# An attention and two-MLP kernel: the up products of tile pairs as seven block products, and the first MLP for all tiles before the second

## The reference, cut to what matters

```
a   = softmax(normed k^T @ normed q / tau)         # 256 x 256, columns normed over 6016 tokens
x   = v @ a                                        # 6016 x 256
g, u = x @ w_gate, x @ w_val                       # 256 -> 1536 each
y   = (silu(g) * u) @ w_out                        # 1536 -> 256
h   = y @ w_in2                                    # 256 -> 2048
out = (h * clip(h + 3, 0, 6) / 6) @ w_out2         # 2048 -> 256
```

## Time and profile before

| what | us |
|---|---|
| median of 3 runs (lowest, highest) | 1154.29 (1154.23, 1155.18) |
| the profiled execution, its own time | 1154.73 |
| its span in the trace | 1152.9 |
| PE busy | 1148.9 |
| DVE, ACT, POOL busy | 711.6, 271.6, 84.2 |

### The profile page before, as it was taken

One profiled execution on the slowest core, in us unless ns is written; L12 is line 12 of the kernel. 1 busy time (PEld: TensorE's weight loads), 2 busy tenths in 40 slices (PEclk: granted clock), 3 DMA queues, 4 the chain that ended last, 5 costly groups with the idle time before them and its releaser, 6 DMA issues.

```text
span 1152.9 us, 14602 instructions
## 1 busy us (share of the span) xinstructions
PE 1148.9 (100%) x5190; PEld 962.1 (83%) x5190; DVE 711.6 (62%) x1174; ACT 271.6 (24%) x453; POOL 84.2 (7%) x54
## 2 busy tenths in 40 slices
PE   9999999999999999999999999999999999999999
PEld 7888888888888888888888888888888888888998
DVE  6786854764664575574485476466557447548557
ACT  7721211211211221221121121122122122112122
POOL 7993000000000000000000000000000000000000
PEclk9999999999999999999999999999999999999999
DMA  9641020020010002002002002001100200100100
GB/s 380 213 143 41 1 37 0 0 36 0 0 21 15 0 0 36 0 0 36 0 0 36 0 0 36 0 0 18 18 0 0 36 0 0 32 0 0 19 1 15
DMA packets 105185, 33.77 MB, mean 29 GB/s; under 512 B 95569, under 2 KB 99537, under 8 KB 105169
## 3 DMA queue, kind: packets, MB, share of 16 engines
q1 hardware_dynamic: 104592, 32.38, 11.2%
q10 hardware_dynamic: 576, 1.18, 0.3%
HBM read 27.39 MB, written 6.16 MB: 29 GB/s over the span
## 4 chain that ended last, share of the span: by engine, by line
PE 99%; DMA 0%; DVE 0%; issue 0%
PE psum L842 33%; PE psum L865 32%; PE psum L853 22%; PE psum L877 5%; PE psum L721 2%; PE psum L825 1%; PE psum L895 1%; PE psum L753 1%; PE psum L734 0%; PE psum L893 0%; DMA qk_first<-in_k 0%; PE psum L909 0%; PE psum L787 0%; PE psum L892 0%; PE psum L800 0%; PE psum L809 0%
## 5 line engine op out<-in xcount | busy, mean ns | idle before, releaser
L865 PE MATMUL psum<-prod,down_w 128*128 128x512 f32 (+1 forms) x1644 | 410.2, 387 | 0.0
L865 PEld LDWEIGHTS psum<-prod,down_w 128*128 128x128 f32 x1644 | 307.9, 188 | 61.6
L853 PE MATMUL psum<-yT,up_w 128*128 128x512 f32 (+1 forms) x1152 | 281.7, 385 | 0.0
L853 PEld LDWEIGHTS psum<-yT,up_w 128*128 128x128 f32 x1152 | 215.3, 188 | 41.8
L668 DVE TENSOR_TENSOR act_out<-psum,act_out 128x512 f32<-128x512 f32 (+1 forms) x144 | 97.9, 680 | 235.3 <-PE psum L842 235.3
L842 PE MATMUL psum<-vT,gate_w 128*128 128x512 f32 (+1 forms) x864 | 215.4, 384 | 0.0
L842 PE MATMUL psum<-vT,val_w 128*128 128x512 f32 (+1 forms) x864 | 215.4, 384 | 0.0
L478 ACT ACTIVATE act_out<-psum 128x512 f32<-128x512 f32 (+1 forms) x144 | 85.1, 591 | 470.5 <-PE psum L842 444.0
L842 PEld LDWEIGHTS psum<-vT,gate_w 128*128 128x128 f32 x864 | 161.4, 188 | 30.9
L842 PEld LDWEIGHTS psum<-vT,val_w 128*128 128x128 f32 x864 | 161.4, 188 | 30.8
L681 DVE SCALAR_TENSOR_TENSOR act_out<-act_out,psum 128x512 f32<-128x512 f32 (+1 forms) x192 | 129.2, 673 | 77.0 <-ACT act_out L486 76.9
(11 more groups left out here) (102 smaller groups left out, 373.2 us busy)
## 6 DMA issues: line engine op xcount, KB each, us to landing
out<-out_sb SPq DMA_DIRECT2D x45, 128.0 KB, 2.5
v_in<-in_v SPq DMA_DIRECT2D x44, 128.0 KB, 3.3
qk<-in_q SPq DMA_DIRECT2D x8, 512.0 KB, 9.1
qk<-in_k SPq DMA_DIRECT2D x7, 512.0 KB, 10.7
w_stage<-in_moe_w_out SPq DMA_DIRECT2D x7, 512.0 KB, 3.9
w_stage<-in_moe_w_in SPq DMA_DIRECT2D x4, 512.0 KB, 3.7
qk_more<-in_q SPq DMA_DIRECT2D x3, 512.0 KB, 11.4
qk_more<-in_k SPq DMA_DIRECT2D x3, 512.0 KB, 12.2
```

The source lines that it names most:

```text
L853: end = mm(HID[j % 4][:, 0:n], up2_w[:, part, b, j * P:(j + 1) * P], yT[:, m, b, 0:n], start=(part, m, b) == (0, 0, 0), stop=(part, m, b) ...
L865: end = mm(banks[h][:, 0:n], w[:, part, j, h * P:(h + 1) * P], prod[:, c % 4, m, 0:n], start=j == 0 and (part, m) == PASSES[0], stop=False)
```

## The change

The 11 full tiles are no longer treated alike. Tile 0 and the 384-token tile stay alone and keep the old products (`first_alone`, `second_alone`). Tiles 1 to 10 form five pairs (left and right). For a pair and a pair of weight rows (gate and value block j in the first MLP; hidden blocks 2w and 2w + 1 in the second) the up products are a 2 x 2 by 2 x 2 product of blocks: 8 block products before, now 7, of sums and differences of blocks, with sums of results afterwards. One such step is a *frame*; the code calls it f. The first MLP has 5 x 12 = 60 frames (0 to 59), the second 5 x 8 = 40 (60 to 99); u or w is the number of a frame in its pair.

- The seven inputs of a pair (`x_even`, `x_odd`) need four differences (`sum_x`, POOL), seven casts to the high part (`cast_x`, ACT, one frame after another) and seven low parts (`split_x`, POOL).
- In a frame PE makes products 0 to 6 (numbered as in the code): 0, 3, 4, 5 go into one chain of sums in one PSUM bank, 1 and 6 into the right tile's, 2 into the left tile's. ACT copies the chain's state to SBUF after products 0, 3 and 4 (`kept1`, `kept6`, `kept7`), and DVE adds the bank of the right or left sums to those copies. The down products, 12 in a frame of the first MLP and 24 in one of the second, stand between products 3, 4 and 5.
- The seven weights are formed by POOL: for the first MLP after the fold (`join_up`, `sum_up`), for the second during the fifth pair of the first MLP (`split_up2`, `split_down2`), where the first MLP's weights are overwritten.
- The order over the tiles changes: first MLP for all tiles, then the second. y goes to a DRAM tensor `y_rows` and comes back (`keep_left`, `keep_right`, `load_y`). All loops are written out.

The core of the diff:

```diff
+    PAIRS = TILES // 2
+    FRAMES1, FRAMES2 = J1, J2 // 2
+    SECOND = PAIRS * FRAMES1
+    FRAMES = SECOND + PAIRS * FRAMES2
...
+            load_y(0)
+            keep_left(PAIRS - 2)
+            keep_right(PAIRS - 2)
+            for n, src in enumerate(PIECES2):
+                if n == 0:
+                    sp.wait_ge(v_read, KC * (TILES + 1))
+                else:
+                    sp.wait_ge(w2_split, n)
+                sp.dma_start(stage2, src).then_inc(w2_loaded, 16)
+            load_y(1)
...
+                summed(1, 4, 0)
+                pool.wait_ge(x_summed, 4 * pair + 1)
+                summed(3, 6, 1)
+                summed(4, 6, 4)
+                pool.wait_ge(x_summed, 4 * pair + 2)
+                summed(5, 2, 3)
...
+            def split_x(pair):
+                for k in range(7):
+                    pool.wait_ge(x_high, 7 * pair + k + 1)
+                    high, low = (XS[pair % 2][:, k, part, :] for part in range(2))
+                    nc.gpsimd.tensor_tensor(low, raw_x(pair, k), high.bitcast(fp32), ALU.subtract).then_inc(x_ready, 1)
...
+                pool.wait_ge(w2_loaded, 16 * (n + 1))
+                pool.wait_ge(p3_summed, frames_before(PAIRS - 1) + 2 * n + 2)
...
+                at = {k: issued(nc.gpsimd.tensor_copy(high[k], source[k])) for k in range(7)}
+                for k in range(7):
+                    pool.wait_ge(w2_step, at[k])
+                    issued(nc.gpsimd.tensor_tensor(low[k], source[k], high[k].bitcast(fp32), ALU.subtract))
...
+            sum_x(PAIRS)
+            for n in range(UP2_PIECES):
+                split_up2(n)
+            split_x(PAIRS)
+            for n in range(DOWN2_PIECES):
+                split_down2(n)
+            for pair in range(PAIRS + 1, 2 * PAIRS):
+                sum_x(pair)
+                split_x(pair)
...
+            def cast_x(pair, k):
+                act.wait_ge(x_summed, 4 * pair + 4)
+                nc.scalar.copy(XS[pair % 2][:, k, 0, :], raw_x(pair, k)).then_inc(x_high, 1)
...
+                nc.scalar.copy(kept1(f), chain(f)).then_inc(p1_kept, 1)
+                if f > 0:
+                    high_first("L", f - 1)
+                    high_first("R", f - 1)
...
+                nc.scalar.copy(kept6(f), chain(f)).then_inc(p6_kept, 1)
+                if 4 <= u <= 10:
+                    cast_x(pair + 1, u - 4)
...
+                nc.scalar.copy(kept7, chain(f)).then_inc(p7_kept, 1)
+                if u == 1 and pair > 0:
+                    keep_y_left(pair - 1)
+                act.wait_ge(row2_right, f + 1)
+                nc.scalar.activation(kept7, kept7, ACT.Silu).then_inc(gate_right, 1)
+                act.wait_ge(p4_summed, f + 1)
+                if f > 0:
+                    act.wait_ge(low_of["L"], f)
+                nc.scalar.activation(gated_left, chain(f), ACT.Silu).then_inc(gate_left, 1)
...
+                relu("1L", f)
+                if g > 0:
+                    high_second("1R", f - 1)
+                high_second("1L", f)
+                if pair + 1 < 2 * PAIRS:
+                    for k in X_CASTS.get(w, ()):
+                        cast_x(pair + 1, k)
...
+            def first_frame(f):
+                pair, u = f // FRAMES1, f % FRAMES1
+                if f > 0:
+                    add_row1_right(f - 1)
+                    gate_first(f - 1)
+                add_row1_left(f)
+                if f > 0:
+                    low_first(f - 1)
+                if u == 2 and pair > 0:
+                    keep_y_right(pair - 1)
+                if u in TURN_AT and pair + 1 < PAIRS:
+                    if f == TURN_AT[0]:
+                        dve.wait_ge(y_alone_stored, 64)
+                    turn_x(pair + 1, TURN_AT.index(u))
+                add_row2_right(f)
...
+            def second_frame(f):
+                g = f - SECOND
+                pair, w = PAIRS + g // FRAMES2, g % FRAMES2
+                if g == 0:
+                    add_row1_right(f - 1)
+                    gate_first(f - 1)
+                else:
+                    clip("2L", f - 1)
+                    add_row1_right(f - 1)
+                    low_second("2R", f - 1)
+                if g == 1:
+                    keep_y_right(PAIRS - 1)
+                add_row1_left(f)
+                if w == 1 and pair > PAIRS:
+                    turn_out(pair - 1, 1)
+                if g == 0:
+                    low_first(f - 1)
+                else:
+                    clip("1R", f - 1)
+                    low_second("2L", f - 1)
+                clip("1L", f)
+                if g > 0:
+                    low_second("1R", f - 1)
+                low_second("1L", f)
+                add_row2_right(f)
+                clip("2R", f)
+                if w == 0 and pair > PAIRS:
+                    turn_out(pair - 1, 0)
...
+                if u == 0:
+                    pe.wait_ge(x_ready, 7 * pair + k + 1)
+                for part, m in PASSES:
+                    end = mm(bank, w[:, u, k, part, :], XS[pair % 2][:, k, m, :],
+                             start=start and (part, m) == PASSES[0], stop=stop and (part, m) == PASSES[-1],
+                             skip_group_check=not start)
...
+                    if f >= 2:
+                        down_first(f - 2, half)
+                elif f == SECOND:
+                    for side in range(2):
+                        down_first(SECOND - 2 + half, side)
+                else:
+                    for x in ORDER2[2 * half:2 * half + 2]:
+                        down_second(f - 1, x)
+            def frame(f):
+                if f == 0:
+                    pe.wait_ge(prod_full, 2 * J1)
+                if f < FRAMES1 and f % 4 == 0:
+                    pe.wait_ge(up_sum_ready, 4 * (f // 4 + 1))
+                if SECOND <= f < SECOND + FRAMES2 and f % 2 == 0:
+                    pe.wait_ge(w2_split, (f - SECOND) // 2 + 1)
+                if f >= 2:
+                    pe.wait_ge(row1_right, f - 1)
...
+                product_of(f, 0, chain(f), start=True, stop=True).then_inc(p1_summed, 1)
+                if f >= 1:
+                    pe.wait_ge(row1_left, f)
+                product_of(f, 1, right_sums(f), start=True, stop=True)
+                if 1 <= f <= SECOND:
+                    pe.wait_ge(gate_left, f)
+                elif f > SECOND:
+                    pe.wait_ge(full["2L"], f - SECOND)
+                product_of(f, 2, left_sums(f), start=True, stop=True).then_inc(p2_summed, 1)
+                pe.wait_ge(p1_kept, f + 1)
+                product_of(f, 3, chain(f), stop=True).then_inc(p6_summed, 1)
+                downs_of(f, 0)
+                pe.wait_ge(p6_kept, f + 1)
+                product_of(f, 4, chain(f), stop=True).then_inc(p7_summed, 1)
+                downs_of(f, 1)
+                pe.wait_ge(p7_kept, f + 1)
+                product_of(f, 5, chain(f), stop=True).then_inc(p4_summed, 1)
+                pe.wait_ge(row2_right, f + 1)
+                product_of(f, 6, right_sums(f), stop=True).then_inc(p3_summed, 1)```

PE, in the middle of the first MLP. Before, two hidden blocks of one tile:

```order
L842 MATMUL psum<-vT,gate_w 128x512 [waits prod_full]
L842 MATMUL psum<-vT,gate_w 128x512 x5
L842 MATMUL psum<-vT,val_w 128x512 x6
L865 MATMUL psum<-prod,down_w 128x512 [waits prod_high]
L865 MATMUL psum<-prod,down_w 128x512 x3
L863 REGISTER_ALU
L865 MATMUL psum<-prod,down_w 128x512 [waits prod_ready]
L865 MATMUL psum<-prod,down_w 128x512
L842 MATMUL psum<-vT,gate_w 128x512 [waits prod_full]
```

More of the change, by code:

```diff
@@ L230, in attention_mlp_mlp_kernel @@
-        MLP2_AT = len(PIECES)
-        second = zip(up_pieces(w_in2, up2_w, F2), down_pieces(w_out2, down2_w, J2))
-        PIECES += [piece for pair in second for piece in pair]
-        def staged(n):
-            a = PIECES[n][2]
-            return w_stage[:, n % 2, :].rearrange("p (a c) -> p a c", a=a)
+        down_view = w_out.rearrange("(j p) c -> p j c", p=P)
+        PIECES = [(down_view[:, j:j + 4, :], down_w[:, j:j + 4]) for j in range(0, J1, 4)]
+        up2_view = w_in2.rearrange("(k p) n -> p k n", p=P)
@@ new lines, in _ @@
+            pool.wait_ge(fold_ready, len(GROUPS_OF_FOLD))
+            for n in range(UPS):
+                join_up(n)
+            for n in range(UPS - 1):
+                sum_up(n)
+            sum_x(0)
+            split_x(0)
+            sum_up(UPS - 1)
+            for pair in range(1, PAIRS):
+                sum_x(pair)
[6 more added lines that the diff above has]
+                split_down2(n)
@@ L386, in _ @@
+            for pair in range(PAIRS + 1, 2 * PAIRS):
+                sum_x(pair)
+                split_x(pair)
+            for i in range(2):
+                for b in range(KC):
+                    pool.wait_ge(y_alone_high, KC * i + b + 1)
+                    high, low = (XS[i][:, 2 * b, part, 0:alone(i)] for part in range(2))
```

(35 more changed lines are left out.)

809 lines of the change are left out of this document (610 added, 199 removed).

## The result

| | median us | lowest, highest |
|---|---|---|
| before (4 runs) | 1154.38 | 1154.23, 1155.18 |
| changed (4 runs) | 1127.10 | 1126.15, 1127.42 |

A forecast was written before the change was run, and what follows sets the result against it. PE, busy throughout, was taken to bound the kernel. The terms, -68.0 + 4 + 8 + 7 + 20 + 8 + 3 + 2, sum to -16 us, giving 1138 us; forecast 1115 to 1150 (0.54), whole range 1100 to 1158.

The forecast's parts named there:

- Term 1: All 100 frames: three fewer matmuls each, 300 in all at 0.2267 us, 68.0 us off.
- Term 2: Frame u = 2: DVE's copies of the last pair's right sums delay right down products; +4 us (0 to 7).
- Term 3: First MLP, u = 4: POOL's input subtractions delay DVE's two multiplications, five times; +8 us (2 to 13).
- Term 4: Frames 0 and 1: without down products between, PE waits for each copy; +7 us (4 to 10).
- Term 5: Frames 51 to 62: POOL's chain of weight splits, loads and differences ends late for PE; +20 us (3 to 25).
- Terms 6 and 7: Second MLP, w = 0, 1: POOL's differences delay DVE, +8 us (0 to 15); output transposes delay down products, +3 (0 to 5).
- Term 8: Joints between frames and lone tiles: +2 us (0 to 6).
- The layout of a frame: Quiet frames: handoffs covered, PE never waits; 7.48 us in the first MLP, 10.2 in the second.
- Rival 2: Frame loop through DVE and ACT does not fit, PE waits every frame; slower, 1181 us; chance 0.09.
- The wait that decides: Frame 62: PE's longest wait, 8 us or more, for ACT's copy, with ACT waiting for POOL's sum_x.
- Rival 1: The cover holds: DVE mostly escapes POOL, multiplications stay near 0.69 us; 47 us off, 1107; chance 0.30.
- Rival 3: Change of weights takes longer: POOL loses more per turn and loads share queues with y; +40, 1158 us; chance 0.07.

The follow-up runs named there:

- eight_products: Changed kernel with product 5 of each frame made twice, restoring the three removed matmuls per frame: 1184.32 us.
- late_casts: Changed kernel with ACT's seven casts of pair 6's inputs moved to frames 64 to 67, from 62 to 67: 1119.32 us.
- two_stages: Changed kernel with second and fourth pieces of w_in2 loaded into y_right, so that loads run beside POOL's splits: 1118.18 us.
- memset_sums: Changed kernel with POOL's four input differences replaced by memsets of the same outputs from pair 1 on: 1118.49 us.
- three_edits: Changed kernel with early_right, sums_on_dve and two_stages together: 1109.61 us.
- three_thin: three_edits with the 32 POOL subtractions that make low parts of w_in2, the second MLP's up weights, replaced by memsets: 1105.89 us.
- early_right: Changed kernel with keep_y_right in frame u = 2 placed before DVE's addition of the left sums: 1123.63 us.
- sums_on_dve: Changed kernel with input differences from pair 1 on moved from POOL to DVE, some casts later and one y load earlier: 1119.89 us.

## Why the prediction was right, and where not

| step | forecast | measured |
|---|---|---|
| Term 1, 300 matmuls | -68.0 | -68.0: 4890 in the trace, quiet frames 7.48 |
| Term 2, `keep_y_right` | +4 | 3.1: four waits of 0.7, one of 0.3 |
| Term 3, `sum_x`, first MLP | +8 | 6.6: 1.29, 1.29, 1.30, 1.30, 1.43 |
| Term 4, frames 0 and 1 | +7 | 5.4: 0.83, 0.84, 2.40, 0.84, small ones |
| Term 5, change of weights | +20 | 19.3, of it 1.6 by the clock behind frame 62's wait |
| Terms 6 and 7, `sum_x` and the output | +8, +3 | 3.8 together |
| Term 8, joints | +2 | 0.6 |

Term 5 is the rest of frames 48 to 67 (7.8 + 13.9) without the 1.4, 0.7 and 0.3 that belong to terms 3 and 2. About 1 us in frames 0 to 47 has no place in the table: the matmuls right behind each wait start another 0.11 late or less.

**The layout of a frame** was right: quiet frames lose nothing in either MLP. Rival 2 (the loop does not fit) did not happen; eight_products does not bear on it.

**The wait that decides** was right in its place, its cause and nearly its size: 7.74 where "8 us or more" was forecast. The chain of POOL from the first piece on, reckoned as 96.0 of work and loads and 19.5 of turns, 115.5, measured 111.5 (542.62 to 654.13): the turns cost 16 and not 19.5. late_casts, two_stages and memset_sums each shorten it or move its end, and each makes the wait in frame 62 smaller or takes it away.

**A wait that it did not name** is the one of 4.6 ahead of frame 60, for the low parts of pair 5, with 1.5 more in that frame: the prediction had only "short waits in frames 51 to 60". It follows from its own terms. The first low part is ready 2.3 + 45.2 + 11.7 (three loads) + 13.5 + 1.2 = 73.9 after the start of frame 51, and PE is there at 67.3; measured, 72.7. The sum is not touched, because POOL sets the end in frame 62 all the same.

**Where it was wrong: terms 6 and 7**, 7 of the 11 us between forecast and result. The step was "about 4 operations wait 1 us each". In the trace POOL's differences start at 714.79, when y has landed, and hold one or two of DVE's by 1 us each; in the stretch before PE's wait DVE turns the output, which reads PSUM and is not held (1.30 for two):

```profile
714.79 4.35 POOL L626 TENSOR_TENSOR x_odd_raw<-x_odd_raw 128x512 f32<-128x512 f32 x3 [8.01 <-DMA x_odd_raw<-y_rows]
...
718.03 1.66 DVE L1209 SCALAR_TENSOR_TENSOR slots<-slots 128x512 f32<-128x512 f32 x1 [0.70 <-ACT slots L884]
...
719.61 1.30 DVE L1224 STREAM_TRANSPOSE out_sb<-psum 128x512 f32<-128x512 f32 x2
```

memset_sums puts the differences' own part at 1.5 us (0.68 and 0.87 gone); the output's is 0.5 in each of four pairs. I had given each pair the price of u = 4 without laying it out for that frame, and the 2.6 us a pair do not follow from the step either: 4 us of delay less 2.6 to 3 of slack are 1 to 1.4 a pair, 3 to 4 in all, where 8 were put down. The rest is terms 2, 3, 4 and 8, each a little too high: these four add up to 5 us.

**The clock** was taken at nothing, because the rows of before had only full speed. PE lost 3.5 us by it in the profiled execution, but the sum feels only the 1.6 behind the wait in frame 62: the 1.9 in frame 60 would otherwise have been waited for in frame 62 (reckoned, not tried). Its upper bound was also miscounted: a frame of the second MLP has 45 matmuls, not 51, so 10.2 us. The Trainium skill (TensorE: Matmul & The Clock Gate, "What's actually happening") says that an idle TensorE falls to 1.2 GHz and comes back only after work; the trace agrees (0.50 in 652 to 658). late_casts, which removes the wait, removes the half clock behind it. That term 5 came out near 20 nevertheless is in part luck: up to product 5 of frame 62 the trace has 17.7 us more than the matmuls alone (the prediction's layout gave 21.7), and the clock added 1.6.

**Rival 1** (the cover holds, 1107) was wrong in what it said of POOL: the multiplications' means are 805 and 841 ns, not 690. On terms 3 and 5 it was far off (2 and 3 against 6.6 and 19.3), on term 6 nearer than the forecast (0 against 1.5). **Rival 3** (term 5 at 40, 1158) did not happen.

## What to carry to other kernels

When matmuls are saved and their work goes to other engines, lay out one quiet step and then each irregular step by itself: the quiet ones were free, and the whole loss came from a few frames in which a copy, a cast or a side chain stood ahead of what the tensor engine needed. Work placed on GpSimd is paid for in VectorE's two-input operations beside it, so its place matters more than its amount; moving it to VectorE helped where GpSimd was idle, and not beside GpSimd's splits. A side chain that is too long shows as one long wait far from it, and the first thing to try is to move the instruction that waits for it behind the one that the tensor engine waits for: that alone gave 8 us here.

## What the runs showed of the hardware

**The same wait, two clocks.** In frame 1, at 160 us, every version of the changed kernel has a wait of PE of 2.4 us (eight_products 1.8). In 7 of the 11 profiled executions the granted clock then fell, in 4 (the changed kernel, memset_sums, three_edits, three_thin) it did not. The changed kernel has 4.51 for the 18 matmuls behind it, two_stages this:

```profile
160.05 0.96 PE L1538 MATMUL psum<-x_even,up_w 128*128 128x512 f32 x3 [2.23 <-ACT slots L860]
161.68 5.99 PE L1538 MATMUL psum<-x_even,up_w 128*128 128x512 f32 x18 [0.68 <-ACT slots L866]
```

That is 1.5 us by itself, nearly half of what early_right is worth. It may be a part of why runs of one kernel lie up to 4.2 us apart here (memset_sums 1115.62 to 1119.84) and those of before less than 1. The record speaks both ways: in three_edits two runs with a mean granted clock of 1.000 took 1106.24 and 1106.90 and three with 0.997 took 1109.61 to 1110.08, but in the changed kernel the two with 0.991 were no longer (1126.15, 1126.91) than the two with 0.995 (1127.28, 1127.42). It is a reason to read an edit's worth from the stretch that it touches. Of the other long waits, all of 4.4 us and more were followed by half clock, and so were one of 2.9 (sums_on_dve) and one of 2.35 (three_thin); one of 2.04 (memset_sums) and the two of 1.7 and 1.9 in two_stages were not.

**GpSimd's casts and VectorE.** POOL's cast of 1024 columns takes 1.04 when alone and about 1.5 beside DVE (644.99, as in the earlier trace rows). A memset beside DVE is another matter. In three_thin seven memsets lie over two of DVE's operations with two SBUF inputs, which take 1.28 us as they do alone:

```profile
564.76 1.83 POOL L681 MEMSET up_w<- 128x256 f32 x7
565.18 1.28 DVE L1045 TENSOR_TENSOR prod<-slots,prod 128x512 fp32r<-128x512 f32 x2
```

The Trainium skill (SBUF — State Buffer, "SBUF: two separate sides") says that a DVE operation with two SBUF inputs is blocked only by a GpSimd operation that reads SBUF; a memset reads nothing, and the trace agrees: 1.28 here, against 3.59 for two beside POOL's split in sums_on_dve.
